# The sum T3 of the next block's features placed after the fourth rest of gates, and a weight pair loaded one product earlier

## The reference

```python
x = attention(q, k, v)                    # 4 x 8 heads x 576 x 64 -> 2304 tokens x 512
def layer(x, w_in, w_out, g):             # w_in 512 x 2048, w_out 2048 x 512
    h = x @ w_in
    return (h * (1.0 / (1.0 + np.exp(-g * h)))) @ w_out
x = layer(x, moe_w_in, moe_w_out, 1.0)
out = layer(x, moe2_w_in, moe2_w_out, 1.702)
```

## Time and profile before

| | |
|---|---|
| median of 3 runs | 848.26 us |
| lowest and highest | 846.18 and 851.70 us |
| profiled execution | 845.45 us |
| its span, first to last instruction | 843.7 us |
| PE busy | 816.2 us, 97% of the span |
| DVE busy | 667.5 us, 79% |
| ACT busy | 533.9 us, 63% |
| POOL busy | 207.5 us, 25% |
| DMA | 205.37 MB, mean 243 GB/s |

### The profile page before, as it was taken

The page is one execution under the profiler, slowest core; times in us unless marked ns, Lnnn a source line. Parts: engine busy times, 40 slices in busy tenths (PEclk is TensorE's granted clock), DMA queues, the critical chain, the costliest instruction groups (busy, mean ns, idle before and its releaser), DMA issues.

```text
span 843.7 us, 15737 instructions
## 1 busy us (share of the span) xinstructions
PE 816.2 (97%) x5691; PEld 787.6 (93%) x5691; DVE 667.5 (79%) x959; ACT 533.9 (63%) x847; POOL 207.5 (25%) x215
## 2 busy tenths in 40 slices
PE   7997988999999999999999999999999999999998
PEld 4776767999999999999999999999999999999998
DVE  6889895989999878888967888899865678655465
ACT  4676765567754667846567755578555677466663
POOL 5778787742005532015510000000000000000000
PEclk9999899999999999999999999999999999999999
DMA  5676556757867778768887777878787878887773
GB/s 173 196 217 187 155 182 219 270 177 280 261 221 245 266 260 316 255 211 267 275 283 251 234 248 258 258 246 279 239 306 248 273 255 266 266 273 256 277 260 127
DMA packets 98312, 205.37 MB, mean 243 GB/s; under 512 B 8416, under 2 KB 56032, under 8 KB 98240
## 3 DMA queue, kind: packets, MB, share of 16 engines
q1 hardware_dynamic: 98240, 204.42, 73.5%
HBM read 160.87 MB, written 43.52 MB: 242 GB/s over the span
## 4 chain that ended last, share of the span: by engine, by line
PE 77%; DVE 10%; DMA 4%; POOL 4%; issue 3%; ACT 1%; SPq 1%; POOLq 0%; DVEq 0%; ACTq 0%
PE hid L309 41%; PE yp L332 35%; DMA qk<-in_qkT 4%; DVE gr L482 2%; DVE wh L284 2%; DVE sums L1010 1%; POOL pband L889 1%; DVE xs L245 1%; DVE smb L1034 1%; POOL vpair L898 1%; POOL pavg L893 1%; PE pt L1084 0%; PE po L1149 0%; DVE mxb L1022 0%; POOL vavg L902 0%
## 5 line engine op out<-in xcount | busy, mean ns | idle before, releaser
L309 PE MATMUL hid<-xs,wh 128*128 128x384 f32 x2016 | 352.5, 334 | 1.6 <-DVE hw L462 1.2
L309 PEld LDWEIGHTS hid<-xs,wh 128*128 128x128 f32 x2016 | 349.2, 188 | 4.1 <-issue 3.5
L332 PE MATMUL yp<-gr,wh 128*128 128x384 f32 x2016 | 350.9, 334 | 1.8 <-DVE gr L482 1.8
L332 PEld LDWEIGHTS yp<-gr,wh 128*128 128x128 f32 x2016 | 349.5, 188 | 2.3 <-issue 2.3
L275 ACT ACTIVATE wh<-wr 128x1024 fp32r<-128x1024 f32 (+1 forms) x164 | 164.6, 1003 | 155.1 <-PE hid L309 119.5
L482 DVE TENSOR_TENSOR gr<-G,gr 128x768 fp32r<-128x768 f32 x144 | 138.8, 974 | 47.8 <-ACT gr L382 47.8
L382 ACT ACTIVATE gr<-G 128x768 fp32r<-128x768 f32 x144 | 121.7, 845 | 68.7 <-PE yp L332 67.4
L284 DVE TENSOR_TENSOR wh<-wr,wh 128x1024 fp32r<-128x1024 f32 x76 | 90.0, 1185 | 21.6 <-ACT wh L275 21.6
L349 ACT ACTIVATE G<-G 128x1152 f32<-128x1152 f32 x48 | 55.7, 1161 | 0.0
L457 DVE TENSOR_TENSOR hv<-p,hid 128x384 f32<-128x384 f32 x48 | 26.4, 550 | 26.9 <-PE hid L309 21.3
L245 DVE TENSOR_TENSOR xs<-x,xs 128x768 fp32r<-128x768 f32 x42 | 42.9, 1022 | 5.8 <-ACT xs L241 5.8
(11 more groups left out here) (88 smaller groups left out, 824.7 us busy)
## 6 DMA issues: line engine op xcount, KB each, us to landing
wh<-rests SPq DMA_DIRECT2D x72, 512.0 KB, 3.8
wr<-sums_out SPq DMA_DIRECT2D x48, 512.0 KB, 4.9
wr<-in_w_out SPq DMA_DIRECT2D x36, 512.0 KB, 5.2
rests<-wh SPq DMA_DIRECT2D x36, 512.0 KB, 3.3
wr<-sums_in SPq DMA_DIRECT2D x40, 384.0 KB, 4.0
wr<-in_w_in SPq DMA_DIRECT2D x40, 256.0 KB, 3.5
qk<-in_qkT SPq DMA_DIRECT2D x16, 576.0 KB, 6.0
G<-in_w_in SPq DMA_DIRECT2D x12, 512.0 KB, 4.4
```

Of the source, the lines that this page charges most:

```text
L309: last = eng.matmul(hid[:, at, 0:HALF], lhsT=wh[:, w % SLOTS, part, a % 4, cc * P:(cc + 1) * P], rhs=xs[:, rest, q, cc, :], start=start an ...
L332: last = eng.matmul(yp[:, at + m, 0:HALF], lhsT=wh[:, w % SLOTS, part, p % 4, m * P:(m + 1) * P], rhs=gr[:, p, rest, :], start=start and p ...
```

## The change

It does two things. The sum T3 of the next block's features leaves `prepare_x` (DVE, i = 0, a == 2) and is issued after `rest_gates(n, 1, 3)` (same i, a == 3), before the second weights' rest of that i. And the pair 8 n + 9 is loaded in `batch` at k = 26 instead of k = 28, for n = 0 and n = 1.

```diff
@@ -260,7 +260,7 @@
             if n == N:
                 return
             rest_x(eng, n, FILLS[i])
-            for q in {B11: (T1, T3), T1: (T2,), B21: (T4,)}.get(FILLS[i], ()):
+            for q in {B11: (T1,), T1: (T2,), B21: (T4,)}.get(FILLS[i], ()):
                 sum_x(eng, n, q)
 
         def round_weights(eng, w):
@@ -528,6 +528,8 @@
                         elif i == 4:
                             for b in range(1, 4):
                                 sum_t4(n, b)
+                        elif i == 0 and n + 1 < N:
+                            sum_x(eng, n + 1, T3)
                 if i == 6:
                     results(n)
                 rest_weights(eng, w + 1 + SLOTS)
@@ -659,7 +661,7 @@
                             load_pair(8 * n + p + 1)
                 elif n < 2 and k == 17:
                     load_pair(8 * n + 8)
-                elif n < 2 and k == 28:
+                elif n < 2 and k == 26:
                     load_pair(8 * n + 9)
                 load_batch(w + RAWS + 1)
                 if k == 1 and n:
```

## The result

The changed kernel takes 852.46 us (median of 22 runs, 849.52 to 856.65) against 849.10 for the kernel before (22 runs, 845.94 to 852.15). The ratio is 1.0038, with a 95% interval of 1.0027 to 1.0049, so by the ratio it is 3.2 us slower (the two medians differ by 3.4). That is within 1%, and clear of no change.

What follows compares the result with a forecast made beforehand. PE was taken as the bound, with DVE the bound in block 0's second half. Part 1's 0 plus 0.8 (block 0) and 0.4 (block 1) gave +1.2 us on 848.26: 849.5 us, range 845.0 to 853.5.

Steps and rivals of the forecast that it cites:

- rival B: SP's stand delays landings in blocks 0 and 1, at 250 GB/s: +5 us, 853; range +2.5 to +7, chance 0.16.
- signs of being wrong: Wait before product 6 gone, wait inside block 1 smaller, or PE idle in the middle of block 1's product 6.
- PE loses little, so no large gain or loss: Feed-forward part: PE loses only 6.1 us, 0.7% of the time, so a gain over 1% isn't there.
- Part 1 costs 0: Block 0's DVE work: T3 and a rest of gates trade places, nobody waits for either, 0 us.
- The pair's load stands at the T4 sums; nobody gains: SP's queue at k = 26: SP waits until 243.4, pair comes 4.4 us earlier, nothing gained at SP.
- Block 0, the landings: Batches 30 and 31 land late, DVE waits 0.2 to 1.6 us in all, passed on to PE.
- Block 0, contention: POOL's additions meet other DVE work in block 0; stretch changes by +0.6 to -1 us.
- Block 1: Rest of batch 29's late landing costs 0 to 0.1 us, batch 31's chain 0 to 0.8; taken as +0.4.
- Rival A: Block 0's end: POOL's additions leave the results and PE's waits shrink, 844.8 us at most; chance 0.14.
- The fit by bytes: Block 1: 2 us plus bytes at 436 GB/s lands everything by 367.2, before ACT's 367.92, so price 0.

Runs made afterwards that it cites:

- e9: Against the kernel before: pair load at k = 26 in block 0 only, with SP also waiting for the second rest of product 6's gates; ratio 1.0069.
- e1: Against the kernel before: only T3 summed later, after the fourth rest of gates, pair load unmoved; 849.06 us, ratio 0.9995.
- e3_load_block0: Against the kernel before: pair load moved to k = 26 in block 0 only; 850.29 us, ratio 1.0007.
- e8: Against the kernel before: pair 8 n + 8 loaded at k = 15 behind that step's raw load, instead of k = 17; 848.21 us, ratio 0.9980.
- e3b: The same program as e3_load_block0, measured again against the kernel before; 851.21 us, ratio 1.0027.
- e7: Changed kernel plus 24 small matmuls issued while PE waits just inside block 1; 852.16 us, ratio 1.0041 against the kernel before.
- e5: Against the kernel before: SP waits for the T4 sums at k = 26, pair still loaded at k = 28; 850.93 us, ratio 1.0022.
- e6: Against the kernel before: pair loaded at k = 26 in blocks 0 and 1, but behind that step's raw batch load; 847.77 us, ratio 0.9987.
- e2: Against the kernel before: only the pair load moved to k = 26 in blocks 0 and 1, T3 unmoved; 852.89 us, ratio 1.0034.

## Why the prediction was right, and where it wasn't

The forecast was +1.2 us, the measured change +3.2, inside the range and within 1%. The direction and the place were right. The size was well under, and by its own table the result fell into rival B (+2.5 to +7), to which I gave 0.16. One of the signs of being wrong came too: PE idle in the middle of block 1's product 6. That the time still lies in the range is because the range took in most of B. The 849.5 us themselves stood on a median of 3 runs, 848.26; on the 849.10 of 22 the same working gives 850.3.

- **PE loses little, so no large gain or loss.** Right: the kernels made from parts of the change stay within 0.4% of before, and e9 within 0.7%.
- **Part 1 costs 0.** Right, 0.9995 (e1). The fourth rest was not late, DVE stays dense, and T3 took the stretch beside POOL (1.49 us).
- **The pair's load stands at the T4 sums; nobody gains.** Right. It was issued 0.07 us behind them, and the batches behind it.
- **Block 0, the landings.** This is the first term that was mis-sized, and the step that failed: a bound from one trace. I bounded batch 30's last piece by 5.1 us and batch 31's by 5.5; they took 5.4 and 6.2. The bound of 5.5 came from the same 1.97 MB, issued within 2.7 us too, which had landed 8.2 us after the first issue. Now it took 251.82 + 6.2 - 249.01 = 9.0 us in block 0, and 371.78 + 6.3 - 369.07 = 9.0 in block 1. What differs is that more was issued right behind (the store of a rest at 252.97 and batch 32 at 253.77, or batch 62 at 372.33), while before nothing followed for 4 us. That this traffic slowed the transfers ahead of it isn't shown, and the spread between executions is as large: the six transfers of the earlier trace rows, in the old order with nothing behind, had all landed 7.9, 8.7, 8.8, 8.8 and 8.8 us after the first issue in e3_load_block0, e8, e1, e3b and e9, the last piece after 5.2 to 6.1 us. In the new order it was 8.7 to 9.1 us in block 0 (six traces) and 8.3 to 9.6 in block 1 (five). So the 5.5 us were one draw from a spread that reaches 6.1. DVE waited 1.33 + 0.78 = 2.1 us where I had 0.2 to 1.6.
- **Block 0, contention.** I took it as about even. It fell: POOL worked partly in the holes that DVE now had, and its stretch of DVE went from 1.5 us to 0.5 in the profile. That gave back 0.8 of the 2.1 us, which is why PE's stretch grew by 1.3 (1.1 to 1.3 in the four profiles with this part, 1.2 on average). So +0.8 was low by 0.4.
- **Block 1.** I had 0 to 0.1 us for the rest of batch 59 and 0.4 in all through batch 31. It was the other way round: the rest landed 6.2 us after its issue instead of 3.6 to 5.5 and PE idled in the middle of product 6: 0.4 to 1.1 us more in five executions, 0.8 on average. Batch 31 hardly added to that in four of them (0.03 to 0.06 us at the next boundary), but 1.2 us in e7's, where its last piece took 6.9 us. e5, where batch 59 was on time, lost 1.3 us by the same chain.
- **The clock.** I had no term for it. In three of the five profiles with the longer wait the granted clock then stood at half for some 3.4 us, 1.6 to 1.9 us more for PE. The waits alone are 1.2 + 0.8 = 2.0 us, with 0.3 for the next boundary on average over the five; with three fifths of 1.7 for the clock it is 3.3, against 3.2 measured. That the sum comes out is no proof: five profiles can't settle either share, e7 recovered nothing, and its waits alone made 3.0 us. How much of the 3.2 us is the clock's is open.
- **Rival B** had the right mechanism at too high a price. It took 250 GB/s as the mean of these halves, where the earlier trace rows show 256 and 275, and needed 9.4 us for the burst; 9.0 were measured. DVE's wait in block 0 was 2.1 us where B had 2.7, and block 1 lost 1.0 on average where B had 2.1.
- **Rival A** (POOL's additions leave the results and PE's waits shrink) has e6 against it: they left, and the waits stayed.
- **The fit by bytes.** The Trainium skill's fit (SBUF — State Buffer, section "The DMA setup-cost knee") would have had 0 for block 1. The 9.0 us measured for 1.97 MB, where the estimate by the fit is 6.5, speak against using it for a queue of several transfers.

## What to carry to other kernels

A load that can wait on a semaphore should stand in its queue behind the transfers that are needed sooner: one line's order was worth the whole loss here (1.0034 in e2, 0.9987 in e6). When a chain has no slack, take the bound for a late landing from several executions and not from one (the same burst landed in 7.9 to 8.8 us here), and look at PE's clock behind a longer wait. A step moved on an engine that is busy without a hole changes nothing unless someone waits for what passes it.

## What I had not expected of the hardware

- The same program with the same wait of PE (2.31 and 2.28 us) had the granted clock at 1.00 behind it in one execution and at half for 3.4 us in the other, which took 1.6 to 1.9 us. Behind a wait that grew by 1.1 us the loss can thus be more than that growth, and it isn't so each time.
- Transfers that landed in 3.6 to 4.1 us at the head of such a burst or apart from one took 6.1 to 6.3 us near the end of 1.97 MB issued within 3 us, even the last of them, of 128 KB only.
- A POOL addition of 128 x 256 that takes 0.74 us alone took 2.85 us beside DVE's dense subtractions (the changed kernel, at 253.29), while the DVE instructions beside it took their usual 0.95. Later it is DVE's L284, at 258.88, that was stretched (1.45 instead of 0.95). So either of the two can be the one that pays. The Trainium skill (SBUF — State Buffer, section "Who interferes with whom") calls the shared ports an exclusive lock and has the order of issue decide who blocks. The rows fit the lock, but the order only in part: the L245 and L482 at 253.73 and 254.60 started after the addition and took their usual 0.95, and in e6 an addition that began at 249.66 took 3.62 us in the same way. So the time lost in such an overlap may fall on the engine that has slack.
